# One table for the preparation of weights and tokens, and another order of second products, in a Strassen-Winograd feed-forward kernel

## What is computed

```python
qn = q / (np.linalg.norm(q, axis=1, keepdims=True) + 1e-06)      # k alike
s = kn.transpose(0, 2, 1) @ qn / tau                             # 256 x 256
a = np.exp(s - s.max(-1, keepdims=True))
a /= a.sum(-1, keepdims=True) + 1e-09
x = (v @ a)                                                      # 6016 x 256
h = x @ w_in1;  x = (h - np.tanh(h)) @ w_out1                    # layer 1
h = x @ w_in2;  out = np.where(h > 0.0, h, np.exp(np.minimum(h, 0.0)) - 1.0) @ w_out2
```

## Time and profile before

| | |
|---|---|
| median of 3 runs | 1047.57 us (1046.94 to 1048.36) |
| the profiled execution | 1048.32 us, span of its instructions 1046.5 us |
| TensorE busy with matmuls | 1029.9 us, 98% |
| VectorE busy | 822.6 us, 79% |
| ScalarE busy | 764.0 us, 73% |
| TensorE's granted clock | 0.998 of full, mean |

### The profile page before, as it was taken

One profiled execution on the slowest core, in us unless ns is written; L12 is line 12 of the kernel. 1 busy time (PEld: TensorE's weight loads), 2 busy tenths in 40 slices (PEclk: granted clock), 3 DMA queues, 4 the chain that ended last, 5 costly groups with the idle time before them and its releaser, 6 DMA issues.

```text
span 1046.5 us, 13719 instructions
## 1 busy us (share of the span) xinstructions
PE 1029.9 (98%) x4556; PEld 855.7 (82%) x4556; DVE 822.6 (79%) x1378; ACT 764.0 (73%) x1360; POOL 0.8 (0%) x7
## 2 busy tenths in 40 slices
PE   8989999999999999999999999999999999999997
PEld 6847788888888888888997788888888888888996
DVE  5779877767776776777887987887887887787775
ACT  6576767666766767667778887878777787877874
POOL 0000000000000000000000000000000000000000
PEclk9999999999999999999999999999999999999999
DMA  9932003003002101002113002101101201200202
GB/s 357 294 63 41 1 1 81 1 1 79 2 1 59 18 1 41 1 15 96 54 52 102 1 1 61 20 1 50 32 1 41 41 1 36 41 1 0 41 1 36
DMA packets 117558, 46.24 MB, mean 44 GB/s; under 512 B 100336, under 2 KB 108528, under 8 KB 117232
## 3 DMA queue, kind: packets, MB, share of 16 engines
q1 hardware_dynamic: 113344, 43.99, 15.8%
q10 hardware_dynamic: 4144, 1.38, 0.6%
HBM read 33.03 MB, written 12.32 MB: 43 GB/s over the span
## 4 chain that ended last, share of the span: by engine, by line
PE 88%; DVE 5%; ACT 4%; issue 2%; DMA 1%; ACTq 0%; DVEq 0%
PE r_ps L313 15%; PE r_ps L315 14%; PE r_ps L314 14%; PE x_ps L313 6%; PE x_ps L314 5%; PE x_ps L315 5%; PE z_ps L313 4%; PE z_ps L315 4%; PE z_ps L314 4%; PE x_ps L320 2%; PE q_ps L320 2%; PE y_ps L314 2%; PE y_ps L315 2%; PE y_ps L313 2%; PE q_ps L314 2%
## 5 line engine op out<-in xcount | busy, mean ns | idle before, releaser
L553 ACT ACTIVATE g_hi<-g 128x512 fp32r<-128x512 f32 (+1 forms) x384 | 236.6, 616 | 157.0 <-DVE g L763 69.7
L633 DVE TENSOR_TENSOR g_lo<-g,g_hi 128x512 fp32r<-128x512 f32 (+1 forms) x384 | 259.8, 677 | 55.6 <-ACT g_hi L553 46.5
L313 PE MATMUL r_ps<-g_hi,w_out_hi 128*128 128x512 f32 (+1 forms) x768 | 296.8, 386 | 3.4 <-issue 2.5
L315 PE MATMUL r_ps<-g_hi,w_out_lo 128*128 128x512 f32 (+1 forms) x768 | 296.3, 386 | 0.0
L314 PE MATMUL r_ps<-g_lo,w_out_hi 128*128 128x512 f32 (+1 forms) x768 | 296.0, 385 | 0.0
L313 PEld LDWEIGHTS r_ps<-g_hi,w_out_hi 128*128 128x128 f32 x768 | 144.3, 188 | 33.2 <-issue 5.8
L315 PEld LDWEIGHTS r_ps<-g_hi,w_out_lo 128*128 128x128 f32 x768 | 144.3, 188 | 27.0
L314 PEld LDWEIGHTS r_ps<-g_lo,w_out_hi 128*128 128x128 f32 x768 | 144.3, 188 | 26.7
L313 PE MATMUL x_ps<-t_hi,w_ops 128*128 128x512 f32 (+1 forms) x288 | 112.9, 392 | 0.5 <-ACT y_ps L533 0.2
L314 PE MATMUL x_ps<-t_lo,w_ops 128*128 128x512 f32 (+1 forms) x288 | 111.3, 386 | 0.0
L315 PE MATMUL x_ps<-t_hi,w_ops 128*128 128x512 f32 (+1 forms) x288 | 111.2, 386 | 0.0
(11 more groups left out here) (107 smaller groups left out, 1476.2 us busy)
## 6 DMA issues: line engine op xcount, KB each, us to landing
v_blocks<-v_dram SPq DMA_DIRECT2D x40, 128.0 KB, 3.1
x_scratch<-side SPq DMA_DIRECT2D x20, 256.0 KB, 2.0
vt<-x_scratch SPq DMA_DIRECT2D x20, 256.0 KB, 3.6
out_dram<-v_blocks SPq DMA_DIRECT2D x80, 64.0 KB, 1.9
k_ring<-k_dram SPq DMA_DIRECT2D x9, 512.0 KB, 8.5
q_ring<-q_dram SPq DMA_DIRECT2D x9, 512.0 KB, 9.4
w_in_sb<-moe_w_in_dram SPq DMA_DIRECT2D x1, 2048.0 KB, 8.8
w_out_raw<-moe_w_out_dram SPq DMA_DIRECT2D x1, 2048.0 KB, 15.3
```

The source lines that it names most:

```text
L313: nc.tensor.matmul(ps, w_hi, m_hi, start=start, stop=False, skip_group_check=True)
L315: return nc.tensor.matmul(ps, w_lo, m_hi, start=False, stop=stop, skip_group_check=True)
L553: nc.scalar.activation(g_hi[b][n % DEPTH[b]][:, 0:width], g[b][:, 0:width], ACT.Copy).then_inc(g_rounded[b], 1)
L633: return nc.vector.tensor_tensor(lo, x, hi.bitcast(F32), ALU.subtract)
```

## The change

1. **Weights of layer 2** (`SUM2`, `PART2`, `PART_OUT2`): one sum and one split of a w_in block per quad where up to two stood, from quad 45 on; the w_out blocks one per quad in quads 45 to 52. The rounding of a block stands in the quad of its sum (`round_w`) or one quad before its split (`round_w_out`, between the copies to `h12` and to `z_ps`).
2. **Weights of layer 1**: the sums of blocks 4 and 5 go from the end of quad 0 to places right before the additions h22 and h12 of that quad. `round_w_out(0)` goes ahead of the tanh of h12, `round_w_out(1)` to quad 1; `split_w_out(0)` goes directly behind the split of g11 in quad 0.
3. **Place of the w_out split on VectorE**: between the splits of g12 and g21 (quads 2 to 7 and 45 to 52), before it was behind both.
4. **Tokens** (`TURNS`, `t_steps`): in pair 0 one transposition each in quads 1 and 2 and two in quad 3, before two each in quads 1 and 2. The five token steps of pairs 1 and 7 come one quad later, in quads u = 4 to 7 and the next pair's u = 0.
5. **Moves** (`move_rows(p - 1, 0, 0)` and `(1, 0)`): in the first quad of a pair round they stand ahead of the rounding of g11, before ahead of that of g22.
6. **Second products**: in the first quad of a pair round the order is 11, 21, 22, 12, before 11, 22, 21, 12. The last quad is written out: P7 and P3 follow P2 at once, then 22 and 12 of quad 94, P4, 22 and 12 of quad 95, then 21 of quad 94, 11 and 21 of quad 95.

```diff
-SUM2 = {2: (0,), 4: (1,), 6: (2, 3), 8: (4, 5), 10: (6, 7)}
-ROUND2_LATE = {2: (0,), 4: (1,), 6: (2,), 8: (4,), 10: (6,), 12: (7,)}
-ROUND_OUT2 = {4: (0,), 6: (1,), 7: (2,), 9: (3, 4), 11: (5,), 12: (6,), 14: (7,)}
...
+SUM2 = {2: 0, 4: 1, 5: 2, 6: 3, 7: 4, 8: 5, 9: 6, 10: 7}
+PART2 = {3: 0, 5: 1, 6: 2, 7: 3, 8: 4, 9: 5, 10: 6, 11: 7}
+PART_OUT2 = {5 + u: u for u in range(QUADS)}
...
-                    order = ("11", "22", "21", "12") if n < ALL else ("22", "12", "11", "21")
+                    order = ("11", "21", "22", "12")
...
+            product(n, P2, Y, False).then_inc(h_ready["11"], 1)
+            pe.wait_ge(z_seeded, n + 1)
+            product(n, P7, Z, False).then_inc(p7_done, 1)
+            product(n, P3, X, False).then_inc(p3_done, 1)
+            second(n - 1, "22")
+            second(n - 1, "12")
+            pe.wait_ge(h_ready["22"], n + 1)
+            product(n, P4, Z, False).then_inc(h_ready["21"], 1)
+            second(n, "22")
+            second(n, "12")
+            second(n - 1, "21")
+            second(n, "11")
+            second(n, "21")
...
+                if moves and u == 0:
+                    move_rows(p - 1, 0, 0)
+                    move_rows(p - 1, 1, 0)
                 round_g(n, "11")
...
                 low(n, "22", h22)
-                low(n, "12", h12)
                 if n == 0:
                     copy_wf(7)
                     round_w_out(0)
-                if n + 1 < QUADS:
+                low(n, "12", h12)
+                if 1 <= n and n + 1 < QUADS:
                     round_w_out(n + 1)
...
+                if 2 <= n < QUADS:
+                    split_w_out(n)
+                if second2(n) in PART_OUT2:
+                    split_w_out(QUADS + PART_OUT2[second2(n)])
                 if n > 0:
                     split_g(n - 1, "21")
...
                 split_g(n, "11")
+                if n == 0:
+                    split_w_out(0)
...
                 split_g(n, "22")
-                if n == 0:
-                    split_w_out(0)
-                    sum_w(4)
-                    sum_w(5)
```

More of the change, by code:

```diff
@@ L76, with t_steps, second2 @@
 ROUND_AFTER = {0: (P2,), 1: (P6,)}
-def t_from(p):
-    return 1 if p == PAIRS else 3
+TURNS = ({1: ((0, 0),), 2: ((0, 1),), 3: ((1, 0), (1, 1))}, {1: ((0, 0), (0, 1)), 2: ((1, 0), (1, 1))})
+def t_steps(n):
+    for p in (n // QUADS, n // QUADS + 1):
+        first = {1: 4, PAIRS: 1, PAIRS + 1: 4}.get(p, 3)
+        step = n - QUADS * (p - 1) - first
+        if 1 <= p < 2 * PAIRS and 0 <= step < 5:
+            yield p, step
+def second2(n):
+    return n - (FIRST2 - QUADS)
 def place(n):
@@ L431, in _ @@
                 product(n, P3, X, False).then_inc(p3_done, 1)
[L432 to L433 removed]
+                between(n, 2)
                 pe.wait_ge(h_ready["22"], n + 1)
                 product(n, P4, Z, False).then_inc(h_ready["21"], 1)
[L436 to L437 removed]
                 between(n, 3)
[L439 to L440 removed]
+            n = ALL - 1
+            pe.wait_ge(h_ready["12"], n)
+            product(n, P1, X, True).then_inc(p1_done, 1)
+            pe.wait_ge(p5_copied, n)
+            product(n, P5, Q, True).then_inc(p5_done, 1)
+            second(n - 1, "11")
+            pe.wait_ge(y_seeded, n + 1)
+            product(n, P6, X, False).then_inc(p6_done, 1)
+            product(n, P2, Y, False).then_inc(h_ready["11"], 1)
[11 more added lines that the diff above has]
+            second(n, "21")
         @block.scalar
@@ L585, in _ @@
                     copy_wf(5)
[L586 to L591, removed]
+                for tp, step in t_steps(n):
+                    for op in ROUND_BEFORE.get(step, ()):
+                        round_t(tp, op)
+                if n == 1:
+                    round_w_out(1)
+                if second2(n + 1) in PART_OUT2:
+                    round_w_out(QUADS + PART_OUT2[second2(n + 1)])
                 act.wait_ge(p6_done, n + 1)
@@ L598, in _ @@
                     copy_wf(6)
+                if moves and u == 0:
+                    move_rows(p - 1, 0, 0)
+                    move_rows(p - 1, 1, 0)
                 round_g(n, "11")
-                for op in ROUND_AFTER.get(u - t_from(p + 1), ()) if prepares else ():
-                    round_t(p + 1, op)
+                for tp, step in t_steps(n):
+                    for op in ROUND_AFTER.get(step, ()):
+                        round_t(tp, op)
                 if 1 <= n and n + 2 < QUADS:
@@ L608, in _ @@
                     round_w_out(0)
-                if n + 1 < QUADS:
+                low(n, "12", h12)
+                if 1 <= n and n + 1 < QUADS:
                     round_w_out(n + 1)
[L611 to L615, removed]
+                if second2(n) in SUM2:
+                    round_w(QUADS + SUM2[second2(n)])
                 round_g(n, "22")
@@ L804, in _ @@
                     sum_w(i)
[L805 to L812, removed]
+                if second2(n) in SUM2:
+                    sum_w(QUADS + SUM2[second2(n)])
+                if second2(n) in PART2:
+                    split_w(QUADS + PART2[second2(n)])
                 if moves and u == 1:
```

48 lines of the change are left out of this document (23 added, 25 removed).

## The result

| | median us | ratio to before, 95% interval |
|---|---|---|
| before | 1047.96 (1046.94 to 1048.78) | |
| changed | 1039.70 (1039.31 to 1040.18) | 0.9922 [0.9905, 0.9939] |

The change takes 8.3 us off, and the forecast was 1039.9, a saving of 7.65 us. The profiled execution of the changed kernel took 1040.18 us with a span of 1038.4, 8.1 us less than the span of before.

What follows compares the result with a forecast made beforehand. TensorE was taken as the bound, losing time to waits. Start 4.9 us saved, second layer 3.1 saved, last quad 0.35 lost: 7.65 off 1047.57 gives 1039.9 us, range 1037.3 to 1043.0.

Steps and rivals of the forecast that it cites:

- The pace as measure: Whole kernel: TensorE's loss read from 0.2267 us a matmul; at most some 13 us to be had, busy time showing less.
- Quad 1: Start of the main loop: a wait of 1.1 us replaces 2.7, half clock goes, the quad then loses 1.45 us.
- Quads 2 to 7: After the first quad: VectorE's preparation mostly fits its room, so of 2.4 us of waits and restarts 0.1 is left.
- Quads 48 to 55: Start of layer 2: earlier moves and lighter preparation leave 0.6 us of 3.70 lost, 3.1 saved.
- Changes of pair: At 11 changes product 21 comes 12 matmuls earlier, its operand 0.6 us early; costed at nothing, bounds 0 and 1.6 saved.
- The last quad: End of the program: TensorE idles 1.6 us, ends 1.05 us later, stores return 0.7; net 0.35 us lost.
- half of that growth: Last quad's stores: landing times grew from 1.8 to 3.1 us through queueing; half, 0.7 us, was given back.
- A: Rival, quad 1 and last quad: idling makes the clock fall; 1041.3 if one wait is enough, 1042.7 if both; 12%.
- B: Rival: work is moved and waits with it, in quads 5, 6 and 50 to 52; 1042.1; 13%.
- C: Rival: the last quad does not wait, its chain starting earlier; 1038.5; 7%.
- D: Rival, slower: product 21 waits at every change of pair, 11 us at 1 us each; 1050.9; 3%.
- E: Rival: something else than w_out held product 11, quad 1 keeps its 4.1 us; 1044.2, or 1046 at worst; 5%.

Runs made afterwards that it cites:

- start undone: Changed kernel with the first w_out pair's rounding and split, the second pair's rounding and sums 4 and 5 in their old places: 1042.42 us.
- the order undone: Changed kernel with second products 11, 22, 21, 12 again in each pair round's first quad, moves of block 0 left early: 1057.20 us.
- the tables undone: Changed kernel with the old tables for the weights of layer 2, moves and orders as changed: 1042.98 us.

## Why the prediction was right, point by point

- **The number.** By the medians 7.65 us were forecast and 8.26 measured; by the two spans it is 8.13. That the times themselves, 1039.9 and 1039.70, lie closer together than the savings is chance: the median of before is 0.4 us higher here than the one the forecast started from.
- **The pace as measure.** Right. Matmuls follow at 0.2267 us where nothing waits, and all of the difference but the 0.09 us ahead of the main loop lies in the places named. In quads 48 to 55 the busy time of TensorE fell by 2.0 us for the same work, 83.36 to 81.37: what looked busy was in part waiting. The idle time of before, 1.37 us, would have bounded the gain at less than half of the 3.12 measured. The Trainium skill (Perfetto Trace Analysis, Identifying the Most-Contended Engine) warns of just this figure; this trace agrees.
- **Quad 1.** Forecast: excess 1.45, a wait of 1.1 at P6, full clock. Measured: 1.53, 1.06, clock 1.00. The copy to y_ps was to end at 74.8 and ended at 74.67. P4 was put at 0.25 and measured 0.13; a restart of 0.11 at the quad's P1, in both kernels, was not in the sum. The half clock of before was put at 1.4 us; by the distances of the starts it cost 1.6, there and with item 2 undone.
- **Quads 2 to 7.** Forecast 0.1, measured 0. By the traces item 4 carries 0.6 us of it (and 0.6 in quad 1), item 3 0.5; the budget of VectorE's work per quad had named 5 and 6 as the fullest, and 5 and 6 wait when one or the other is undone.
- **Quads 48 to 55.** Forecast 3.1 saved, measured 3.12. From the start of quad 49, the copy to y_ps was to begin after 1.89 us, product 22 after 4.5 and z_ps to be there after 5.4; measured 555.26 - 553.37 = 1.89, 4.51 and 5.36. Quad 49 kept 0.54 of the 0.6 us left over, the others nothing.
- **Changes of pair.** Forecast: nothing, the low half of g21 there 3.46 us after the start of the first quad, product 21 at 4.08. Quad 56 of the changed kernel started at 625.31, and VectorE's row is

```profile
628.08 0.69 DVE L660 TENSOR_TENSOR g_lo<-g,g_hi 128x512 fp32r<-128x512 f32 x1 [0.26 <-ACT g_hi L579]
```

  and TensorE's, of product 21,

```profile
629.39 0.39 PE L321 MATMUL r_ps<-g_hi,w_out_hi 128*128 128x512 f32 x1
```

  The first ends 3.46 us after the quad's start, the second begins 4.08 us after it. The second quads of layer 2 kept their waits, 0.37 us in quad 57; those of layer 1 had none to lose. What the prediction did not say is that the order is what the moves' new place rests on; it treated the two as separate edits.
- **The last quad.** The one term that was mis-sized. TensorE's part was right: 1.05 us later, measured 1.02, with a wait of 1.53 where 1.6 was put. The stores gave back 0.95 us where 0.7 was put, "half of that growth". Of the growth from 1.8 to 3.1 us, 0.6 went, so that half was right. What the sum put at nothing is the time from the last matmul to the last issue: 1.53 us instead of 1.87, 0.34 less. Before, eight issues in each of two queues follow each other with 0.05 us or less between them, so the last waits for those ahead of it. In the changed kernel the first four of each queue have been issued by 1032.94, before the last matmul ends at 1033.87, and the other four start at 1033.98. The net loss is 0.07 us, not 0.35. That 0.28 is over half of the 0.48 us between the forecast saving, 7.65, and that of the two spans, 8.13; 0.09 is the main loop's earlier start, and the rest is spread over the other terms.
- **Rivals.** A did not happen: the clock rows at 72.00 and at 1026.00 are 1.00 with waits of 1.06 and 1.53 us in them. The Trainium skill (TensorE: Matmul & The Clock Gate, The HAM clock gate) has the throttled rate as the default that activity lifts; for idling of this length the trace shows no throttling. B did not happen, but its quads 5, 6, 50 and 51 are among those that wait when an item is undone. C did not happen: the last quad waits 1.53 us. D's price is real, 17 us for 1.5 a change; its condition was not met. For E nothing speaks: undoing item 2 brought both pieces of quad 1 back.

## What to carry to other kernels

Measure the bound engine by the distance of its starts, not by its busy time, and then look only at the places where the distance grows; each has one releaser, and the step queued ahead of that releaser is what to move. When a step is moved ahead on an engine that waits in order, ask first which product of another engine it needs: the same early move cost 17 us with one order of TensorE's work and gained 0.35 with the other. At the end of a program, TensorE's last matmul is not the end: idling that spreads the output over time can cost nothing.

## What the runs showed of the hardware

- TensorE's clock fell to half at waits of 2.68 us (kernel before) and 2.66 us (start undone), in each case with some 1.6 us lost. It stayed at 1.00 behind waits of 1.06, 1.41, 1.53 and 1.58 us (quad 1 and the last quad of the changed kernel, product 21 made late, the order undone). No run shows a wait between 1.58 and 2.66.
- The first matmul after a wait costs 0.11 us more with first products and with second products behind a low half of g, 0.08 with second products behind a move.
- In two traces (the start undone, the order undone) the quads of 448 columns of the last pair round took 9.30 us instead of 9.12, every start 0.207 apart instead of 0.203, at a granted clock of 1.00. This is some 1.1 us of each. In three more (the tables undone, order and moves undone, the low half of g11 postponed) the same pace holds in a part of the last quad only, some 0.1 us. Its cause is open, and it can hide a gain of 0.1 us at the end of the program.
